# Routing between attention and the experts: fewer VectorE steps, tables built and multiplied one by one, VectorE's branch turned

## The reference

```python
for s in range(S):
    fresh_e = int(np.argmax(logits[b, s]))
    if s == 0 or local_gate[b, s] < 0.5:
        e = fresh_e
    else:
        e = prev_e if prev_e >= 0 else fresh_e
    prev_e = e
    ...
    h = np.maximum(x[b, s] @ w1[e], 0.0)
    out[b, s] = p[e] * (h @ w2[e])
```

## Time and profile before

| | us |
|---|---|
| median of three runs | 540.93 |
| the profiled execution | 541.39 |
| its span (first to last instruction) | 539.4 |
| TensorE busy (matmul) | 504.4 (94%) |
| VectorE busy | 280.2 (52%) |
| ScalarE busy | 196.4 (36%) |
| Pool busy | 109.7 (20%) |
| mean granted TensorE clock | 0.971 |
| attention, to its last turned-back matmul | 0 to 102.05 |
| routing and first gather | 102.05 to 133.46 |
| experts | 133.46 to 347 |
| mixing | 347 to 539.4 |

### The profile page before, as it was taken

One profiled execution on the slowest core, in us unless ns is written; L12 is line 12 of the kernel. 1 busy time (PEld: TensorE's weight loads), 2 busy tenths in 40 slices (PEclk: granted clock), 3 DMA queues, 4 the chain that ended last, 5 costly groups with the idle time before them and its releaser, 6 DMA issues.

```text
span 539.4 us, 9507 instructions
## 1 busy us (share of the span) xinstructions
PE 504.4 (94%) x3420; PEld 440.0 (82%) x3421; DVE 280.2 (52%) x639; ACT 196.4 (36%) x412; POOL 109.7 (20%) x114
## 2 busy tenths in 40 slices
PE   9899999427999999999999999998999999999997
PEld 9688877317999999999899899986788878888886
DVE  5678887563311414141542531287997685555243
ACT  3988887111011414132423411335444232222010
POOL 3997860002011212122222221000000000000000
PEclk9999999856899999999999999999999999999999
DMA  8554328391510819192992800060000000000012
GB/s 334 209 188 148 112 68 344 120 395 58 186 39 28 353 72 365 61 390 53 398 378 77 363 18 25 19 233 1 0 1 0 2 0 21 19 20 20 21 50 86
DMA packets 19123, 71.12 MB, mean 132 GB/s; under 512 B 2702, under 2 KB 2702, under 8 KB 14864
## 3 DMA queue, kind: packets, MB, share of 16 engines
q1 hardware_dynamic: 16304, 63.93, 31.0%
q0 software_dynamic: 2640, 6.30, 3.3%
q10 hardware_dynamic: 144, 0.44, 0.2%
HBM read 62.53 MB, written 10.49 MB: 135 GB/s over the span
## 4 chain that ended last, share of the span: by engine, by line
PE 78%; DVE 8%; issue 5%; ACT 4%; DMA 4%; SPq 0%; POOLq 0%; POOL 0%; DVEq 0%; ACTq 0%
PE ps L1278 43%; PE ps L1307 20%; PE ps L1171 3%; PE ps L1208 3%; ACT prob L633 2%; DMA w_sb<-in_w_experts 2%; PE ps L1191 2%; PE ps L1134 2%; PE ps L1149 2%; PE ps L1293 1%; PE ps L1370 1%; DVE x_tok L833 1%; DMA x_tok<-y_rows 1%; DMA xin<-x_rows,rows_in 1%; PE ps L1331 1%
## 5 line engine op out<-in xcount | busy, mean ns | idle before, releaser
L1307 PEld LDWEIGHTS ps<-xT,w_sb 128*128 128x128 f32 x1024 | 119.2, 195 | 4.2 <-DVE xT L1027 1.7
L1307 PE MATMUL ps<-xT,w_sb 128*128 128x128 f32 x1024 | 119.8, 279 | 2.2 <-DVE xT L1027 1.5
L1013 DVE SCALAR_TENSOR_TENSOR hT_lo<-ps,hT_hi 128x512 fp32r<-128x512 f32 x32 | 22.1, 690 | 102.5 <-ACT hT_hi L684 102.3
L1022 DVE TENSOR_TENSOR w_lo<-w_sb,w_hi 128x1024 fp32r<-128x1024 f32 x32 | 37.0, 1219 | 39.2 <-ACT w_hi L695 39.2
L1278 PE MATMUL ps<-w_hi,hT_hi 128*128 128x512 f32 x128 | 51.5, 402 | 0.0
L633 ACT ACTIVATE prob<-raw,row_min 128x256 f32<-128x256 f32 (+1 forms) x96 | 45.9, 481 | 11.4 <-DVE row_min L866 11.4
L1278 PE MATMUL ps<-w_hi,hT_lo 128*128 128x512 f32 x128 | 50.1, 391 | 0.0
L684 ACT ACTIVATE hT_hi<-ps 128x512 fp32r<-128x512 f32 x32 | 19.1, 597 | 84.5 <-PE ps L1307 84.5
L1278 PE MATMUL ps<-w_lo,hT_hi 128*128 128x512 f32 x128 | 49.8, 389 | 0.0
L688 ACT COPY yout<-ps 128x512 f32<-128x512 f32 x16 | 9.4, 587 | 85.2 <-PE ps L1278 85.2
L695 ACT CAST w_hi<-w_sb 128x1024 fp32r<-128x1024 f32 x32 | 31.1, 1044 | 12.6 <-DVE slot_part L983 12.6
(11 more groups left out here) (194 smaller groups left out, 950.2 us busy)
## 6 DMA issues: line engine op xcount, KB each, us to landing
w_sb<-in_w_experts SPq DMA_DIRECT2D x32, 1024.0 KB, 9.2
v_sb<-in_vx SPq DMA_DIRECT2D x8, 640.0 KB, 4.0
q_raw<-in_q SPq DMA_DIRECT2D x8, 384.0 KB, 6.0
x_rows<-x_tok SPq DMA_DIRECT2D x2, 1536.0 KB, 8.7
x_tok<-y_rows SPq DMA_DIRECT2D x12, 256.0 KB, 4.8
out_x<-o_sb SPq DMA_DIRECT2D x12, 256.0 KB, 2.0
k_raw<-in_kx SPq DMA_DIRECT2D x7, 432.0 KB, 4.8
wtr<-in_w_tok_rT SPq DMA_DIRECT2D x6, 384.0 KB, 12.3
```

The costliest lines, as they stand in the source:

```text
L1013: dve.scalar_tensor_tensor(hT_lo[:, part, :], ps[:, 1 + half, :].rearrange("p (c q) -> p c q", c=4), 0.0, hT_hi[:, part, :].bitcast(F32), ...
L1022: dve.tensor_tensor(quarter(w_lo, par, q), quarter(w_sb, par, q), w2_hi_quarter(q).bitcast(F32), ALU.subtract).then_inc(s_w2_lo, 1)
L1307: last = pe.matmul(ps[:, 1 + half, f * P:(f + 1) * P], w_sb[:, par, c // 2, j:j + P], xT[:, c, :], start=(c == 0), stop=(c == DC - 1))
```

## The change

- Group 15 (`LAST`) is turned back into bank 3 and waits for the last score operations instead of x of group 14. For groups 14 and 15 VectorE computes reciprocals and logit shares first; their x is written later, group 14's while the codes are transposed, group 15's after the first scan. `add_logits` waits for the share and not for x.
- Codes are made by one comparison and multiplication from `gate_e` (8 minus the expert, so that 0 is free for "hold").
- The last codes of the rows go on a diagonal, and one matmul with the triangular table gives every row the codes of the rows before it, so that one scan over 12 columns and one masked addition fill the holes. One matmul fewer.
- `onehot` is fp32r and so are the two tables (`exact_c`, written by ACT after attention). The counts come first, and the scans read PSUM. Ranks, tiles and slots take fewer operations; place and tile of a slot come from a rounding with a large constant.
- `at_place` is built in 12 operations that hold the token number too, each followed by its own matmul. Empty slots become an index beyond the last row by adding `NO_TOKEN` back. `first_tile` and the gate's sums are written after the tables.
- Pool gathers the first rows straight by a column of `token_at`, before it loads `last_tile`.
- VectorE's branch is on the opposite flag, with `whole_rows()` first and `windows()` second. Pool writes the opposite flag first, and the other engines wait for both.
- TensorE's expert loops are eight loops one behind the other, with bounds loaded before the first rows are turned; the dummy matmuls are 11 after the map and 2 after the first rows.

The diff, cut to its core (removed lines of the routing stand in the listing above):

```diff
@@ -84,11 +86,10 @@
     first[0, ::QT] = 1.0
     put("first", first)
     put("erev", np.tile(E - np.arange(E), NT)[None])
-    put("eone", np.tile(np.arange(E) + 1, NT)[None])
-    put("starts", np.tile(np.arange(NT) * P, E)[None])
+    put("starts", np.tile(np.where(np.arange(NT) > 0, np.arange(NT) * P, -1), E)[None])
     put("carry", np.tile(np.arange(NT) > 0, E)[None])
     put("place", np.arange(P)[None])
-    put("token", p + np.arange(NT)[None] * P + 1)
+    put("token", p + np.arange(NT)[None] * P - NO_TOKEN)
     put("tile", np.tile(np.arange(MAP), NT)[None])
     return t, np.concatenate([rel, np.broadcast_to(np.arange(S)[None], (P, S))], axis=1).astype(np.float32)
@@ -136,6 +137,11 @@
 def prob_home(g):
     return ((0, g - 2), (1, g - 4), (0, g - 2), (1, g - 2), (0, g - 2), (2, g - 6))[g % QT]
+def back_bank(q):
+    return 3 if q == LAST else 7
 def turned_bank(n):
@@ -438,7 +447,7 @@
 def which_path(eng):
-    eng.wait_ge(s_path, 1)
+    eng.wait_ge(s_path, 2)
     return eng.value_load(is_banded[0:1, 0:1], min_val=0, max_val=1)
 def either(eng, band, windows, whole_rows):
@@ -542,7 +551,8 @@
     pool.wait_ge(s_flag, 3)
     pool.tensor_tensor(reach, reach, least, ALU.mult).then_inc(s_flag, 1)
     pool.wait_ge(s_flag, 4)
-    pool.tensor_copy(is_banded[:], reach).then_inc(s_path, 1)
+    pool.tensor_scalar(is_banded[:, 1:2], reach, -1.0, 1.0, ALU.mult, ALU.add).then_inc(s_path, 1)
+    pool.tensor_copy(is_banded[:, 0:1], reach).then_inc(s_path, 1)
     pool.wait_ge(s_one, 1)
     pool.wait_ge(s_mask, 2)
@@ -568,9 +578,13 @@
     pool.wait_ge(s_cleared, 1)
     pool.wait_ge(s_map, 1)
     pool.wait_ge(s_x_out, 16 * B)
+    pool.sem_inc(s_row_in, 1)
+    pool.sem_inc(s_row_seen, 1)
+    last_row = pool.to_reg(TOKENS - 1)
+    pool.indirect_dma_start(xin[:], None, x_rows, bass.IndirectOffsetOnAxis(ap=token_at[:, 1:2], axis=0),
+                            bounds_check=last_row, oob_is_err=False).then_inc(s_m_xin, 16)
+    pool.wait_ge(s_slot_ready, 1)
     last_tile = pool.value_load(first_tile[0:1, E + 1:E + 2], min_val=E - 1, max_val=SLOT_TILES - 1)
-    last_row = pool.to_reg(TOKENS - 1)
     def rows_of(t):
         pool.tensor_copy(rows_in[:], token_at[:, bass.ds(t + 1, 1)]).then_inc(s_row_in, 1)
@@ -675,6 +688,9 @@
     either(act, which_path(act), windows, whole_rows)
+    act.wait_ge(s_c_in, 16)
+    act.copy(exact_c[:].rearrange("p a c -> p (a c)"),
+             cst[:, COL["before"][0]:COL["ones"][1]]).then_inc(s_exact, 1)
     act.wait_ge(s_g_dve, 1)
     act.activation(gate_f[:], gate_e[:], ACT.Exp).then_inc(s_g_act, 1)
     def expert_tile(pair, par, t):
@@ -803,33 +819,40 @@
     dve.wait_ge(s_q_hi, 1)
     dve.tensor_tensor(q_lo[:, 0, :], q_raw[:, 0, :], q_hi[:, 0, :].bitcast(F32),
                       ALU.subtract).then_inc(s_q_split, 1)
...
+    dve.wait_ge(s_path, 1)
+    unbanded = dve.value_load(is_banded[0:1, 1:2], min_val=0, max_val=1)
     def second_half(q):
         dve.wait_ge(s_av, GROUP * (q + 1))
         wait(dve, s_back, q - 1)
         dve.tensor_copy(outT[:, 1, :], ps[:, 6, 0:GROUP * P]).then_inc(s_ot1, 1)
...
+    def shares(q):
         h, half = q // 2, q % 2
         tiles = slice(GROUP * half, GROUP * half + GROUP)
         dve.wait_ge(s_exped, 2 * GROUP * (q + 1))
         sums = den[:, h % 2, tiles, :].rearrange("p i b -> p (i b)")
...
+        if q < LAST - 1:
             dve.wait_ge(s_back, q + 1)
...
+        dve.tensor_tensor(den_e[:, half, :], sums, tiny if q < LAST - 1 else tiny_s[:], ALU.add).then_inc(s_rank, 1)
         dve.wait_ge(s_rank, q + 1)
         dve.reciprocal(rec[:, half, :], den_e[:, half, :]).then_inc(s_den, 1)
...
+    def share_and_back(q):
+        return (rec[:, q % 2, :].rearrange("p (i b o) -> p i b o", i=GROUP, o=1),
+                ps[:, back_bank(q), 0:GROUP * TURNED].rearrange("p (i c) -> p i c", i=GROUP))
+    def logits(q):
+        share, turned_back = share_and_back(q)
+        dve.wait_ge(s_back, q + 1)
         dve.wait_ge(s_den, q + 1)
...
+        dve.tensor_tensor(part[:, q % 2, :].rearrange("p (i b e) -> p i b e", i=GROUP, b=B),
                           turned_back[:, :, P:].rearrange("p i (b e) -> p i b e", b=B),
...
+                          share.to_broadcast([P, GROUP, B, E + 1]), ALU.mult).then_inc(s_part, 1)
+    def rows_of_x(q):
+        share, turned_back = share_and_back(q)
+        h, tiles = q // 2, slice(GROUP * (q % 2), GROUP * (q % 2) + GROUP)
         dve.tensor_tensor(x_tok.rearrange("p (b i) d -> p i b d", b=B)[:, tiles, :, h * DH:(h + 1) * DH],
                           turned_back[:, :, 0:P].rearrange("p i (b d) -> p i b d", b=B),
                           share.to_broadcast([P, GROUP, B, DH]), ALU.mult).then_inc(s_x_done, 1)
@@ -838,12 +861,18 @@
         h, half = q // 2, q % 2
         to = lg.rearrange("p (b i) e -> p i b e", b=B)[:, GROUP * half:GROUP * half + GROUP]
         of = part[:, half, :].rearrange("p (i b e) -> p i b e", i=GROUP, b=B)
-        dve.wait_ge(s_x_done, q + 1)
+        dve.wait_ge(s_part, q + 1)
         if h == 0:
             dve.tensor_copy(to, of).then_inc(s_sum, 1)
         else:
             dve.wait_ge(s_sum, q - 1)
             dve.tensor_tensor(to, to, of, ALU.add).then_inc(s_sum, 1)
+    def normalise(q):
+        shares(q)
+        logits(q)
+        if q < LAST - 1:
+            rows_of_x(q)
     def windows():
         def turned(g):
@@ -908,7 +937,10 @@
                 normalise(g // GROUP)
                 add_logits(g // GROUP)
-    either(dve, banded, windows, whole_rows)
+    with dve.If(unbanded):
+        whole_rows()
+    with dve.Else():
+        windows()
     dve.wait_ge(s_sum, PAIRS // GROUP)
@@ -918,93 +950,86 @@
     def wide(a):
         return a.rearrange("p (n o) -> p n o", o=1).to_broadcast([P, NT, E])
+    def by_tile(a):
+        return a.rearrange("p (n e) -> p n e", n=NT)
+    def by_expert(a):
+        return a.rearrange("p (e n) -> p e n", e=E)
+    def along(a, inner):
+        return a.rearrange("p (n o) -> p n o", o=1).to_broadcast([P, a.shape[1], inner])
+    dve.scalar_tensor_tensor(fresh, lg[:, :, E:E + 1].rearrange("p n o -> p (n o)"), RESET_AT, con("first"),
+                             ALU.is_le, ALU.max)
     then(dve.tensor_reduce(top, lg[:, :, 0:E], AX.X, ALU.max))
     dve.tensor_tensor(gate_e[:], lg[:, :, 0:E], wide(top), ALU.subtract).then_inc(s_g_dve, 1)
...
+    dve.wait_ge(s_g_dve, 1)
+    then(dve.scalar_tensor_tensor(codes[:], gate_e[:], 0.0, by_tile(con("erev")), ALU.is_equal, ALU.mult))
+    then(dve.tensor_reduce(best, codes[:], AX.X, ALU.max))
     dve.tensor_tensor(val, best, fresh, ALU.mult).then_inc(s_p_ready, 1)
+    rows_of_x(LAST - 1)
+    excl = rank_s[:, 0, :]
+    dve.memset(excl[:, 0:1], 0.0)
+    dve.memset(tiles_s[:, 0:NT], 0.0)
     dve.wait_ge(s_row_mm, 1)
...
+    fresh_row = ps[0:NT, 5, 0:P]
+    then(dve.tensor_scalar(hold[:], fresh_row, 0.0, None, ALU.is_equal))
+    then(dve.tensor_tensor_scan(chosen[:], hold[:], fresh_row, 0.0, ALU.mult, ALU.add))
+    ends_at, end_hold, carried = (ends[:, j, :] for j in range(3))
+    dve.tensor_scalar(ends_at, ident[0:NT, 0:NT], chosen[:, P - 1:P], None, ALU.mult).then_inc(s_row_d, 1)
+    rows_of_x(LAST)
     dve.wait_ge(s_row_mm, 2)
...
+    earlier_ends = ps[0:NT, 6, 0:NT]
+    then(dve.tensor_scalar(end_hold, earlier_ends, 0.0, None, ALU.is_equal))
+    then(dve.tensor_tensor_scan(carried, end_hold, earlier_ends, 0.0, ALU.mult, ALU.add))
+    then(dve.tensor_scalar(hold[:], chosen[:], 0.0, carried[:, NT - 1:NT], ALU.is_equal, ALU.mult))
+    dve.tensor_tensor(row[:], chosen[:], hold[:], ALU.add).then_inc(s_row_d, 1)
     dve.wait_ge(s_col_mm, 1)
...
+    dve.tensor_tensor(onehot[:], by_tile(con("erev")), wide(ps[:, 0, 0:NT]), ALU.is_equal).then_inc(s_oh, 1)
+    dve.wait_ge(s_counts, 1)
+    in_tiles, inside = ps[:, 2, 0:E * NT], ps[:, 1, 0:E * NT]
+    rank, slots = rank_s[:, 1, :], rank_s[:, 2, :]
+    then(dve.tensor_tensor_scan(excl[:, 1:], in_tiles[:, 0:E * NT - 1], con("carry")[:, 1:], 0.0, ALU.add, ALU.mult))
+    last_tile_of = slice(NT - 1, NT)
+    then(dve.tensor_tensor(held[:].rearrange("p (e o) -> p e o", o=1), by_expert(excl)[:, :, last_tile_of],
+                           by_expert(in_tiles)[:, :, last_tile_of], ALU.add))
+    needed = rank_s[:, 3, :]
+    then(dve.tensor_tensor(by_expert(needed), along(held[:], NT), by_expert(con("starts")), ALU.is_gt))
+    dve.wait_ge(s_counts, 2)
+    dve.tensor_tensor(rank, excl, inside, ALU.add)
+    then(dve.tensor_tensor_scan(tiles_s[:, NT:], con("ones")[:, 0:E * NT], needed, 0.0, ALU.mult, ALU.add))
+    tiles_to = tiles_s[:].rearrange("p (e n) -> p e n", n=NT)[:, :, NT - 1:NT]
+    then(dve.scalar_tensor_tensor(by_expert(slots), tiles_to[:, 0:E, :].to_broadcast([P, E, NT]), float(P),
+                                  by_expert(rank), ALU.mult, ALU.add))
     dve.wait_ge(s_oh, 1)
     dve.wait_ge(s_g_act, 1)
...
```

(69 more changed lines are left out.)

96 lines of the change are left out of this document (11 added, 85 removed).

## The result

The changed kernel took 538.26 us (median of five runs, 536.47 to 539.36), the kernel before 541.33 beside it; the ratio is 0.9936, interval 0.9914 to 0.9959. Run again with the first experiments it took 538.22 against 542.27, ratio 0.9927 (0.9898 to 0.9956). So it is 3 to 4 us faster, where 7.0 had been forecast: right in direction, outside the range of 530.0 to 537.5. The profiled execution took 539.36, with a span of 537.5.

The account below looks back on a forecast made before the run. The serial 31.4 us between attention and the first expert matmul was taken as the bound; 7.1 + 0.4 - 0.5 = 7.0 us off the profiled 541.39 gave 534.4, or 533.9 from the median 540.93; range 530.0 to 537.5.

Parts of the forecast that it names:

- last logit addition: VectorE at attention's end: it ends at about 101.2 against 103.01, a saving of 1.8 us.
- codes of TensorE: Routing's start: codes ready at 102.5, but TensorE's jump ends at 103.4, losing 0.9 us of the saving.
- map: End of the routing's tables: token map ready at 114.5, against 125.1 before.
- the store landed: Store of x to DRAM, beside the routing: lands at 117.15 against 114.4, 2.6 us after the map.
- Start of the kernel: VectorE's jump moved before attention: code 0 to 1.6 us late, taken as 0.5 us lost.
- Rival 3: Kernel start: code late by 1.6 us instead of 0.5, 535.0; 17% together with rival 2.
- The gather in the load: First gather of rows while expert 1's weights load: 6.0 us taken, between bounds 3.65 and 6.0.
- hand-over: Between map and gather: register load and copy (125.1 to 126.33) go; gather starts at 118.6.
- The first tile: First expert matmul at 126.35 against 133.46, 7.1 us earlier; first 64 expert matmuls 0.4 us shorter.
- Rival 1: Gather not held up, or TensorE keeps 2.4 GHz into the first tile: about 531.5, both 529.1; 22%.
- Rival 2: VectorE still loads code after attention, so the 2.65 us stay: +1.75, 535.6; 17% together with rival 3.
- Rival 4: TensorE loads code entering each written-out expert loop: gain gone from 1.0 us an entry, 547.9 at 2 us; 7%.

Follow-up runs that it names:

- first experiments: Follow-up runs in five rounds beside the kernel before, with the changed kernel run again unaltered as their base: 538.22 against 542.27.
- branch as before: Changed kernel with VectorE's branch put back as before the change (windows code first): 536.1, ratio 0.9887.
- quiet start: Changed kernel with gate weights and far table loaded only after the first score operation: 535.01, ratio 0.9874.
- dummies: Changed kernel with eight more dummy matmuls in TensorE's idle time before the second value matmuls: 535.53, ratio 0.9894.
- thirteen rows of the table: One profiled execution each of the kernel before, the changed kernel (twice) and the follow-up kernels; moments in us from the span's start.
- loops experiment: Changed kernel with TensorE's expert loops as before (four pairs in a loop), first transposes and two dummy matmuls ahead: 537.24, ratio 0.9916.
- last kernel: Changed kernel plus later gate weights and far table, eight dummy matmuls, group 15's x behind group 14's, expert 1's weights after the second gather: 527.54, ratio 0.9747.

## Why the prediction was wrong

The stretch it was about came out as worked. Counted from group 14's turning back, to take the late start out: last logit addition forecast 101.2, found 101.1; codes of TensorE at 103.4, found 103.2, with its jump at 3.80 as its row had it; map 114.5, found 114.7; the store landed at 115.9 (forecast 117.15), after the map, as forecast. The routing's cut is real, 10.4 us up to the map, and most of it was given back outside the routing.

1. **Start of the kernel: the term that failed most.** Forecast 0.5 us, with 1.6 as the worst; it was 3.9. Two mistakes in one step. The jump's price was taken from a row at attention's end, where the DMA engines began to fill only a microsecond after the branch (2.86 us; in "branch as before" 2.9 at a DMA share of 0.01), and used for a place where they were full: there it took 5.8. And what attention does with a late start was left out: TensorE then idled for 2 us instead of 1.15, the granted clock fell, and that added 1.4. The first is shown by the quiet start (3.8 us for the jump). The second is shown in part: the idle time of 1.94 to 1.98 us is in all seven traces with the turned branch and no dummies, but the clock fell in only four of them. So 1.2 to 1.4 of the 3.9 us came with this execution, and 2.9, as in the turned branch in the kernel before, would still be above the worst case of 1.6. Rival 3 had the first mechanism, and its price was too small by more than half.
2. **The gather in the load.** Forecast 6.0, found 7.95 and 7.2. The bound taken was that of one gather issued 8.5 us into a 4 MB load (184.3, load from 175.8). In the same trace a store of 128 result rows, issued at 177.4, took longer (its line, L587):

```profile
DMA to landing us min/median/max: 8.1/8.1/8.1
```

That the load is the cause is shown by putting it later. The store and the hand-over made up for 1.5 us of this.
3. **The first tile** gave 1.5 us instead of 0.4: 8.55 instead of 10.07 for the first 64 matmuls, the granted clock being 0.50 for 2.4 us of them and not for 5. That the dummy matmuls did this is not shown. The kernel before with only its branch turned has none behind the first rows, waited just as long for xT, and gained 1.2:

```profile
133.62 8.87 PE L1312 MATMUL ps<-xT,w_sb 128*128 128x128 f32 x64 [1.53 <-DVE xT L1032]
```

4. **Behind the first tile** 2.1 us were lost that the forecast carried through unchanged: 1.0 up to the last expert tile and 1.1 from there to the end. The chain after waits for weights twice, where single-tile experts meet a load of 13 us:

```profile
251.78 11.32 DMA w_sb<-in_w_experts
...
291.12 1.62 SPq L499
...
292.94 11.03 DMA w_sb<-in_w_experts
```

The kernel before has one such wait in its chain, but TensorE idles at both places in both kernels: 0.20 and 0.48 us before, 0.50 and 1.49 after. The longer ones, before and then after:

```profile
307.18 3.03 PE L1307 MATMUL ps<-xT,w_sb 128*128 128x128 f32 x25 [0.48 <-DMA w_sb<-in_w_experts]
```

```profile
304.20 6.04 PE L1333 MATMUL ps<-xT,w_sb 128*128 128x128 f32 x52 [1.49 <-DMA w_sb<-in_w_experts]
```

SP needed 1.62 us to issue one of the four pieces of that load, where the kernel before needed at most 0.49. The other 1.1 us are the load of the result rows at the head of the mixing stage, again before and then after:

```profile
351.67 3.66 DMA x_tok<-y_rows
```

```profile
348.54 4.79 DMA x_tok<-y_rows
```

Over all thirteen rows of the table the time from the end of the first 64 expert matmuls to the last tile's start lies between 189.6 and 191.5 us (before 190.0, after 191.0), and from there to the end between 205.6 and 207.6 (before 205.9, after 207.0). So the two places are known, but that the change made them longer is not told from scatter, and the cause stays open; undoing the loops did not touch it clearly.

The sum: forecast 126.85 for the first expert matmul (with the 0.5 at the start), found 131.0: 3.4 for the start, 1.95 for the gather, 0.3 for the turning, less 1.5 for store and wake-up. Another 0.95 behind it make 5.1, the distance from 532.4 to the span of 537.5.

Rival 1 (gather not held up) was wrong in this kernel, and became right only when the load was moved. Rival 2 is refuted by the 0.02 us gap. Rival 4, at its price of 7 us and more, is refuted by the loops experiment and by the chain; an effect of a microsecond is not excluded. The chance of faster, 0.91, was right; the range was too narrow: the unknown at the start was bounded by a guess of 1.6 and not by the rows of contended transfers, where a store of rows took 8.1 us under load and 2.8 without.

## What to carry to other kernels

A branch that jumps far has a price that depends on the DMA load beside it (2.9 us here in one place, 5.8 in another): put it where the DMA engines are quiet and another engine is jumping too, and price it by the load at its own place. When a serial stretch is cut, look first for the transfers beside it: here the store of x and the next expert's weights became the bound, and one added wait that held back a load not needed for 40 us gave more (5.0 us by the trace, 6.4 by the medians) than the whole change had (3 to 4). A wait that comes late in a pipeline's start can cost more than its own length: here TensorE idled for 2 us behind it, and in four of seven traces its clock then fell to 1.2 GHz, for 1.2 us more. And a bracket that names a releaser is to be held against the moment at which that releaser was done: in the quiet start it named TensorE, which had been ready for 0.8 us.

## What the runs showed of the hardware

- VectorE's jump over far code, from the branch to the first operation behind it: 5.6 to 6.3 us in seven traces with a mean DMA share of 1.02 to 1.03 over it; 3.8 in the quiet start and 3.7 in the last kernel, at 0.4; 2.9 in the three traces that have it at attention's end. The share over the whole jump is not the whole measure: it was 0.01 in "branch as before" and 0.70 in the kernel before, both 2.9 us. In the latter the load began about a microsecond after the branch, in the quiet start it stopped about a microsecond and a half after it. That the load at the jump's beginning counts fits this, and was not tested.
- TensorE's branch over far code: 3.34 to 3.95 us in thirteen traces, though the DMA share was 0.04 around it in the changed kernel. The two engines are not alike, and why isn't settled.
- The gather of 128 rows of 2 KB: 3.6 to 3.8 us with no load beside it, 7.2 to 8.5 when much of a 4 MB load was still to come, 6.0 when issued 8.5 us into one.
- Twelve operations of 128x128 with two per-partition scalars took 3.16 us, 0.26 each, against 1.68 for one of twelve tiles and against 0.14 to 0.21 that I had put; VectorE set the pace there and not TensorE.
